# Weight splits and one scan moved between VectorE, ScalarE and GpSimd in the first eight slots of a linear-attention and mixer kernel

## The reference

```
state = alpha[t] * state + outer(k[t], v[t]);  y[t] = q[t] @ state          # stage 1, gated linear attention
theta = x @ w_theta;  zr, zi = x * cos(theta), x * sin(theta)               # stage 2, x is stage 1's output
u = x + w_tok_r @ zr + w_tok_i @ zi                                         #   token mix, over 768 tokens
x2 = u + relu(u @ w_ch)                                                     #   channel mix
h = relu(x2 @ w_in);  gate, v = h[:512], h[512:];  v_n = layernorm(v)       # stage 3
out = (gate * (w_spatial @ v_n + b_spatial)) @ w_out
```

## Time and profile before

| | us |
|---|---|
| median of 3 runs | 612.69 |
| lowest and highest of them | 611.33, 613.26 |
| the profiled execution | 611.15 |
| its span, first to last instruction | 609.1 |
| PE busy | 584.8 (96% of the span) |
| DVE busy | 381.5 (63%) |
| ACT busy | 223.4 (37%) |
| POOL busy | 213.1 (35%) |

### The profile page before, as it was taken

How to read it: one execution, slowest core, us unless ns; L and a number is a source line. 1 busy time by engine, 2 the same in 40 slices (tenths; PEclk the granted TensorE clock), 3 DMA queues, 4 the chain that set the end, 5 groups by cost and what they waited for, 6 DMA issues and landing times.

```text
span 609.1 us, 11143 instructions
## 1 busy us (share of the span) xinstructions
PE 584.8 (96%) x4608; PEld 555.9 (91%) x4608; DVE 381.5 (63%) x591; ACT 223.4 (37%) x411; POOL 213.1 (35%) x181
## 2 busy tenths in 40 slices
PE   3798988999999999999999999999999999999998
PEld 3597878999999999999999989999999899989997
DVE  6899785788787887887844257737133713372132
ACT  2555563443343434433444126524132313132110
POOL 4544285442241131421413036437013611362130
PEclk9999998999999999999999999999999999999999
DMA  7852211132151222321323091200220020002002
GB/s 272 286 196 92 66 66 66 66 106 85 48 169 67 76 95 66 105 70 63 105 104 117 0 322 70 77 1 5 74 79 2 1 79 1 1 0 79 1 1 79
DMA packets 20258, 49.53 MB, mean 81 GB/s; under 512 B 1648, under 2 KB 15216, under 8 KB 19696
## 3 DMA queue, kind: packets, MB, share of 16 engines
q1 hardware_dynamic: 20208, 48.81, 23.2%
HBM read 39.37 MB, written 9.44 MB: 80 GB/s over the span
## 4 chain that ended last, share of the span: by engine, by line
PE 83%; DVE 7%; ACT 3%; POOL 2%; issue 2%; DMA 1%; SPq 0%; DVEq 0%
PE psY L436 20%; PE psC L468 6%; PE psY L557 6%; PE psC L418 5%; PE psS L557 4%; PE psF L557 4%; PE psY L534 4%; PE psY L544 3%; PE psF L397 3%; PE psF L524 3%; PE psS L369 3%; PE psY L524 2%; PE psS L534 2%; PE psC L557 2%; PE psS L544 2%; PE psF L544 2%
## 5 line engine op out<-in xcount | busy, mean ns | idle before, releaser
L1032 POOL TENSOR_TENSOR z_lo<-cos_sin,z_hi 128x768 fp32r<-128x768 f32 x23 | 43.1, 1873 | 110.3 <-ACT z_hi L652 110.3
L1098 POOL TENSOR_TENSOR gated_lo<-u_gated,gated_hi 128x384 fp32r<-128x384 f32 x32 | 32.4, 1014 | 123.5 <-ACT gated_hi L758 123.5
L436 PE MATMUL psY<-tok_r_hi,z_hi 128*128 128x384 f32 x141 | 51.4, 364 | 2.7 <-POOL tok_i_lo L1026 1.5
L1019 POOL TENSOR_TENSOR akq<-akq 128x512 f32<-128x512 f32 x23 | 27.4, 1193 | 57.3 <-DVE akq L814 57.3
L436 PE MATMUL psY<-tok_r_hi,z_lo 128*128 128x384 f32 x141 | 47.4, 336 | 0.0
L436 PE MATMUL psY<-tok_r_lo,z_hi 128*128 128x384 f32 x141 | 47.3, 336 | 0.0
L436 PE MATMUL psY<-tok_i_hi,z_hi 128*128 128x384 f32 x141 | 47.3, 336 | 0.0
L436 PE MATMUL psY<-tok_i_hi,z_lo 128*128 128x384 f32 x141 | 47.2, 335 | 0.0
L436 PE MATMUL psY<-tok_i_lo,z_hi 128*128 128x384 f32 x141 | 47.2, 335 | 0.0
L758 ACT ACTIVATE gated_hi<-u_gated 128x384 fp32r<-128x384 f32 x32 | 16.8, 525 | 79.2 <-DVE u_gated L967 79.2
L1039 POOL TENSOR_TENSOR u_lo<-u_f,u_hi 128x384 fp32r<-128x384 f32 x24 | 25.8, 1103 | 47.0 <-ACT u_hi L657 47.0
(11 more groups left out here) (222 smaller groups left out, 1749.6 us busy)
## 6 DMA issues: line engine op xcount, KB each, us to landing
...
```

Source lines behind the costliest of these rows:

```text
L436: mm = pe.matmul(psY[:, j, 0:HALF], Z[s][l][:, q, tile(j)], W[m][:, s, half(h)], start=(s == 0 and q == 0 and n == 0), stop=(s == CHUNKS - ...
L1032: pool.tensor_tensor(Z[c][1][:], trigs[g % 2][:], f(Z[c][0][:]), ALU.subtract).then_inc(z_lo, 1)
L1098: pool.tensor_tensor(GA[1][:, j, half(h)], ug[h][:, j], f(GA[0][:, j, half(h)]), ALU.subtract).then_inc(g_lo, 1)
```

## The change

What it does, slot by slot:

- **Slot 0.** On DVE, `xT_low(0)` and `mask_scores(1)` stand ahead of `decay_queries(2)`, the forward scan of the third chunk. On ACT, `xT_high(0)` stands ahead of the high parts of token pieces 0 and 1.
- **Slot 5.** ACT makes the high parts of pieces 6 and 7 here, ahead of `copy_x(5)`, and not in slot 6. DVE, not POOL, makes their low parts, between `multiply_z(4)` and the angle reduction of chunk 5; they count on a semaphore of their own, `tok_lo_mid`, for which units (1,0) and (1,1) wait.
- **Slot 6.** ACT makes `ch_hi` ahead of `keep_xT(6)`; DVE, not POOL, makes `ch_lo`, after `make_u(0)`.

```
-SPLITS = ((0, 1), (2,), (3,), (4,), (5,), (), (6, 7), (8, 9), (10, 11)) + ((),) * (BATCH * CHUNKS)
+MID_SPLITS = (6, 7)
+SPLITS = ((0, 1), (2,), (3,), (4,), (5,), (6, 7), (), (8, 9), (10, 11)) + ((),) * (BATCH * CHUNKS)
...
                 if k < HALVES:
-                    pe.wait_ge(tok_lo, k * CHUNKS + s // 2 * 2 + 2)
+                    last = k * CHUNKS + s // 2 * 2 + 1
+                    if last in MID_SPLITS:
+                        pe.wait_ge(tok_lo_mid, len(MID_SPLITS))
+                    else:
+                        pe.wait_ge(tok_lo, last + 1 if k == 0 else last + 1 - len(MID_SPLITS))
...
@@ ScalarE, slots 0 to 5
+                if c == CHUNKS - 1:
+                    for i in SPLITS[c]:
+                        tok_high(i)
                 copy_x(c)
-                for i in SPLITS[c]:
-                    tok_high(i)
-                if c == CHUNKS - 1:
+                if c in (0, CHUNKS - 1):
                     xT_high(c)
+                if c < CHUNKS - 1:
+                    for i in SPLITS[c]:
+                        tok_high(i)
                 if c:
                     sines(c - 1)
-                if c < CHUNKS - 1:
+                if 0 < c < CHUNKS - 1:
                     xT_high(c)
...
@@ ScalarE, from slot 6 on
                     xT_high(g)
+                    if g == CHUNKS:
+                        act.wait_ge(ch_in, 16)
+                        act.activation(WC[0][:], raw_ch[:], ACT.Copy).then_inc(ch_hi, 1)
                     keep_xT(g)
...
@@ VectorE, slots 0 to 5
-                mask_scores(c)
+                if c != 1:
+                    mask_scores(c)
...
                 if c == 0:
                     decay_keys(2)
-                    decay_queries(2)
...
                 if c < CHUNKS - 1:
                     xT_low(c)
+                if c == 0:
+                    mask_scores(1)
+                    decay_queries(2)
+            for i in MID_SPLITS:
+                m, pair, cols = tok_part(i)
+                hi, lo = (WR, WI)[m]
+                dve.wait_ge(tok_hi, i + 1)
+                dve.tensor_tensor(lo[:, pair, cols], (raw_r, raw_i)[m][:, pair, cols], f(hi[:, pair, cols]),
+                                  ALU.subtract).then_inc(tok_lo_mid, 1)
...
@@ VectorE, from slot 6 on, behind update_state and make_u
+                    if g == CHUNKS:
+                        dve.wait_ge(ch_hi, 1)
+                        dve.tensor_tensor(WC[1][:], raw_ch[:], f(WC[0][:]), ALU.subtract).then_inc(ch_lo, 1)
...
@@ GpSimd: the same steps removed there
-                    if g == CHUNKS:
-                        pool.wait_ge(ch_hi, 1)
-                        pool.tensor_tensor(WC[1][:], raw_ch[:], f(WC[0][:]), ALU.subtract).then_inc(ch_lo, 1)
```

10 lines of the change are left out of this document (4 added, 6 removed).

## The result

| | before | after |
|---|---|---|
| median of the runs compared, us | 612.01 (4 runs, 610.76 to 613.26) | 606.22 (4 runs, 606.01 to 607.48) |
| ratio, 95% interval | | 0.991 (0.9887 to 0.9932) |
| profiled execution, us | 611.15 | 607.48 |
| its span, us | 609.1 | 605.4 |
| mean granted clock | 0.992 | 0.997 |

The other three runs of the changed kernel have a granted clock of 1.000 and spans of 604.0 to 604.4.

A forecast was written before the change was run, and what follows sets the result against it. DVE was taken to bound slots 3 to 5, and PE, fully busy, everything from slot 9 on. Profiled 611.15 less 3.75 gain plus 1.5 for lower clock gives 608.9; 1.54 for the median gives about 610.4, range 608.4 to 612.3.

The forecast's parts named there:

- delay at (0,4): Slot 5: `z_lo(4)` on POOL waits behind DVE's second split, so PE's unit (0,4) starts 0.8 us late.
- A wait of 1.10 us for `tok_i_lo` ahead of (1,2): Slot 7: pieces 8 and 9, still on POOL, come late, so PE waits 1.3 us ahead of (1,2).
- The price of a stretch: PE running about 3.4 us at the lower clock after a wait costs 1.5 us, give or take 0.3.
- one new stretch: After PE's wait ahead of (0,4) or (1,2), one lower-clock period of about 3.4 us, costing 1.5 us.
- as much above: Median of the changed kernel's runs stands 1.54 us above its profiled execution, as before the change.
- the gain of 3.75 us at (1,4): PE starts unit (1,4) 3.75 us earlier: 3.1 at (1,2) plus the 0.67 us wait gone.
- The waits of slots 6 to 9: PE's shorter waits from unit (1,0) to (1,4), counted as 1.75 us of the gain.
- DVE keeps 0.5 us of the 1.33: Slot 0: first angles come 1.33 us earlier, and 0.5 us of it (bounds 0 to 1.3) reaches slot 5.
- The two meetings with POOL: Slots 1 and 2: piece 2 and `z_lo(0)` on POOL each hold up DVE, two meetings instead of one.
- The first, no new stretch: PE's waits bring no lower-clock period, so all 3.75 us stay: 608.9 us. Chance 0.27.
- the second: Two lower-clock periods, or `z_lo(4)` ahead of DVE's second split; gain 0.7 to 1.2 us, about 611.7. Chance 0.25.
- The third: Late POOL queue meets DVE in each of slots 1 to 5; at 1.3 us per slot, 615.4 us. Chance 0.05.

The follow-up runs named there:

- clean repeat: Changed kernel run again without edit, second group (12 runs); its trace has no period near half clock: 607.72 us, ratio 0.9948.
- The four later groups: Four sets of follow-up runs, each with the kernel before measured on the same chip; its median moved between 610.5 and 611.2 us.
- slot 0 with later pieces: Kernel before plus the slot 0 part, with POOL's low parts of token pieces 2 to 5 one slot later: 608.66 us, ratio 0.9954.
- changed kernel, third: Changed kernel once more without edit, fourth group (6 runs): 608.12 us, ratio 0.9944.
- spread: Changed kernel, POOL's pieces 2 to 5 one slot later, 7 in slot 6, 10 and 11 early in slot 8; 8 and 9 on DVE: 605.52, again 605.98 us.
- the slot 0 kernel: Kernel before with the slot 0 part of the change alone: 611.07 us, ratio 1.000.
- three traces with later pieces: Traces of changed-kernel versions with POOL's pieces 2 to 5 one slot later: that edit alone (607.05, again 607.28 us) or within spread.
- the fillers: Kernel before with unread matmuls put into PE's waits: 611.19 us, ratio 0.9998; the changed kernel with such matmuls: 607.48 us, ratio 0.9943.
- the matmuls at PE's start: Kernel before with 15 unread 128x128 matmuls ahead of PE's first scores: 611.73 us, ratio 1.0013.

## Why the prediction was wrong

**Right, by the rows.** PE's first angles at 18.20 (18.0 said). `z_lo(4)` behind DVE's second split, with 0.64 us of delay at (0,4) (0.8 said). No wait ahead of the first channel mix, at 90.39 and in the clean repeat, the one without a stretch, 3.55 us earlier than before (3.1 said). `u_lo` done at 88.4 (88.1 said). A wait of 1.10 us for `tok_i_lo` ahead of (1,2) (1.3 said). None ahead of (1,4). The splits and `ch_lo` covered. From the start of (1,4) to the end it is 491.6 to 491.8 us in every trace, so what PE has gained there is carried to the end, as said. The price of a stretch was right as well: 1.54 us behind the first channel mix (1.5 said) and 1.26 behind (0,4) (1.5, give or take 0.3). The direction, and the place where the gain is made, hold.

**The step that failed: from the profiled execution to the typical one.** The forecast put one new stretch into the typical execution ("I expect one of the two to bring a stretch", 1.5 us), and the median "as much above" the profiled execution as before, 1.54 us. The profiled execution did have this stretch, yet the other three had a clock of 1.000 and none, and the median came out 1.26 us below the profiled one. That is 2.8 us of the error. The 1.54 us had been read from three executions. The four later groups have 84 executions of the kernel before, with medians of 610.5 to 611.2, so none stands more than 0.1 us above the 611.15 of the profiled one; no run shows the term. The absence of the stretch in three of four was partly luck: over all 22 executions of the changed kernel 11 have a clock below 1.000. Where their stretches lie is known for two of them, both at (0,4). By the Trainium skill ("TensorE: Matmul & The Clock Gate", "Part 1: The HAM clock gate") how many matmuls of the same kernel run at the lower level varies from run to run; the traces of this case agree (0.50 and 1.00 at the same wait of 2.18 and 2.19 us).

**The term that was too small: the gain of 3.75 us at (1,4).** The traces take it apart. Between DVE's mask of slot 5 and PE's (1,4) the time depends on the order of work and on a stretch alone:

| execution | mask of slot 5 | (1,4) | between | stretch there |
|---|---|---|---|---|
| before | 58.85 | 117.46 | 58.61 | at the first channel mix |
| slot 0 with later pieces (slots 5 to 9 as before) | 58.67 | 115.74 | 57.07 | none |
| after | 57.94 | 113.75 | 55.81 | at (0,4) |
| changed kernel, repeat | 58.25 | 112.80 | 54.55 | none |
| changed kernel, third | 57.75 | 113.61 | 55.86 | at (0,4) |
| pieces 6 and 7 on POOL | 58.91 | 115.99 | 57.08 | at (1,0) |
| spread | 57.23 | 110.59 | 53.36 | none |

So the gain of the profiled execution is 0.91 (slot 0) + 2.52 (57.07 - 54.55, the shorter waits) + 1.54 (the old stretch gone) - 1.26 (the new one) = 3.71 us. The forecast had 0.5 + 1.75 + 1.5 - 1.5 = 2.25. The waits of slots 6 to 9 were the largest miss, 0.8 us: half of it is there at the first channel mix, and half comes after it, where pieces 8 and 9 were to hold up (1,2) for longer than they did.

*What DVE keeps in slot 0.* "DVE keeps 0.5 us of the 1.33": the masks show 0.91, 0.60 and 1.10 us in three traces. Part of this spread is the start, where DVE idles 0.20 us before and 0.49, 0.71 and 0.30 us in these traces for a transfer. Its first mask starts at 11.62, 11.95 and 11.46, against 11.41 before, and counted from there DVE keeps 1.12 to 1.15 us in all three. The two meetings with POOL came, but the scan of 27.65 got through before `z_lo(0)` (1.22 us instead of 2.25), and only L818 paid (2.14 us), a meeting that takes the place of the old one at 28.98 and isn't a second one. (The stretches of the kernel before at 29 and at 59.7 us are gone in the profile after too, though PE still waits 1.50 us ahead of 58.08. The forecast had kept them; as DVE is the bound there, they cost nothing either way.)

**The sum again.** Forecast 611.15 - 3.75 + 1.5 + 1.54 = 610.4. With 4.66 and without a stretch: 606.5, and 606.2 came out. So of the 4.2 us of error 0.9 is the gain, 1.5 the stretch that most executions didn't have, and 1.8 the distance of the median from the profiled execution. Over the 12 runs of the repeat the median was 607.72, 2.7 us below the forecast. It stood 1.33 us above the profiled execution, near the forecast's 1.54 by chance only: that execution was of the quick kind. As a gain on the kernel before in the same group, the repeats have 2.7 to 2.8 us between the medians and 3.2 to 3.4 by the ratios, not far from the 2.3 forecast. The range was too narrow as well: its lower end, 608.4, took in no more than 3.75 us of gain and kept the 1.54 in full, though the bound of slot 0 was given as 1.3 us, 0.8 above the value taken.

**The rivals.** The first, no new stretch, was the nearest in its mechanism; its 608.9 misses by 0.9 us of gain and by the 1.8 us of the median. Of the second, neither half came in a trace of the changed kernel: `z_lo(4)` never got in ahead of the splits. Two stretches can't be ruled out in executions without a trace, where the clock is 0.994. The third described a real thing in the wrong number: a late POOL queue does meet DVE anew, but in slot 1 alone, and only in some executions. There it takes slot 0's whole lead: the mask of slot 5 is at 59.13 in the slot 0 kernel and at 58.91 with pieces 6 and 7 on POOL, POOL being first in both, and at 57.23 to 57.52 in three traces with later pieces and no half-rate start.

**Which part pays.** The splits without slot 0 bring 2.8 us. Slot 0 on top brings something only when the multiply of slot 0 comes ahead of POOL's piece 2: 0.6 to 1.1 us at the masks, and 0.35 us between the medians of the two kernels (608.07 and 607.72), which is within their noise. Of the splits, either move does most of the work. With pieces 6 and 7 on DVE and `ch_lo` on POOL nothing is lost (ratio 0.9948). With `ch_lo` on DVE and the pieces on POOL the ratio is 0.9957, and the table gives 57.08 - 1.54 = 55.54 us without its stretch (7.10 us from (1,0) to the channel mix, against 5.56 after): 1.5 of the 2.5 us. In both, the `u_lo` are no longer late and PE's wait ahead of the first channel mix is gone.

**What stays open.** The kernel before has spans from 610.5 to 611.7 beside its usual 607.4 to 609.6, and neither the fillers nor the matmuls at PE's start removed them. Slot 1's race is a candidate, since its multiply already takes 1.30 us in the profile of before, but no trace of such an execution was had. Which of the upper kinds of the changed kernel come from the half-rate start and which from the meeting in slot 1 is open too, and so is why a stretch follows a wait in one execution and not in the next.
